# Chunked delta-rule attention, soft MoE and a gated layer in one kernel: the two halves of a chunk issued side by side

## The reference, cut to what matters

```python
# B, H, S, D = 4, 8, 768, 48
k_n = k / (norm(k) + 1e-6); state = zeros((B, H, D, D))
for t in range(S):
    y[t] = q[t] @ state
    v_old = k_n[t] @ state
    state = state + beta[t] * outer(k_n[t], v[t] - v_old)
# x = y as (B*S, H*D) = 3072 x 384
logits = x @ phi; d = softmax over tokens; c = softmax over slots
slot_out = relu((d.T @ x)[e] @ w1[e]) @ w2[e]        # 8 experts, 4 slots each
x = c @ slot_out
h = x @ w_in; out = (h * sigmoid(1.702 * h)) @ w_out  # 384 -> 2048 -> 384
```

## Time and profile before

| | us |
|---|---|
| median of 3 runs | 526.88 |
| their range | 525.96 to 527.99 |
| the profiled execution | 527.37 |
| its span, first to last instruction | 525.5 |
| TensorE busy | 456.1 (87%) |
| VectorE busy | 353.0 (67%) |
| ScalarE busy | 311.8 (59%) |
| mean granted clock of TensorE | 0.958 |

### The profile page before, as it was taken

One profiled execution on the slowest core, in us unless ns is written; L12 is line 12 of the kernel. 1 busy time (PEld: TensorE's weight loads), 2 busy tenths in 40 slices (PEclk: granted clock), 3 DMA queues, 4 the chain that ended last, 5 costly groups with the idle time before them and its releaser, 6 DMA issues.

```text
span 525.5 us, 17657 instructions
## 1 busy us (share of the span) xinstructions
PE 456.1 (87%) x7296; PEld 335.6 (64%) x7296; DVE 353.0 (67%) x1177; ACT 311.8 (59%) x711; POOL 8.2 (2%) x20
## 2 busy tenths in 40 slices
PE   7548877878777788876999599999999999999997
PEld 4434655656555566554433277788888888888885
DVE  3798999999989986422651377656565666556653
ACT  2212788788878888777230356655655655655553
POOL 2000000000000000000000000000000000000000
PEclk9557899999999999989999799999999999999999
DMA  4911344666531233699999600010100100100101
GB/s 168 374 45 41 95 124 143 190 186 186 159 100 34 78 98 111 178 212 230 335 401 412 239 0 1 7 54 1 60 0 0 60 0 0 60 0 0 62 0 61
DMA packets 24295, 59.18 MB, mean 113 GB/s; under 512 B 3104, under 2 KB 11296, under 8 KB 23840
## 3 DMA queue, kind: packets, MB, share of 16 engines
q1 hardware_dynamic: 24224, 58.16, 34.6%
HBM read 53.43 MB, written 4.72 MB: 111 GB/s over the span
## 4 chain that ended last, share of the span: by engine, by line
PE 53%; ACT 20%; DVE 16%; issue 7%; DMA 3%; ACTq 0%; DVEq 0%
PE bank L815 10%; PE bank L817 10%; PE bank L816 10%; ACT zb L827 9%; PE bank L524 6%; ACT nv L870 4%; DVE tmp L1104 4%; DVE tt L1109 4%; PE bank L793 3%; DMA wo<-in_w_out 2%; DVE g_l L1316 2%; DVE g L1313 2%; PE bank L672 2%; ACT state L827 2%; ACT g_h L827 2%
## 5 line engine op out<-in xcount | busy, mean ns | idle before, releaser
L815 PE MATMUL bank<-g_h,wo_h 128*128 128x512 f32 x288 | 113.0, 392 | 2.3 <-DVE g_l L1316 2.1
L1316 DVE TENSOR_TENSOR g_l<-g,g_h 128x512 fp32r<-128x512 f32 x96 | 66.5, 693 | 71.5 <-ACT g_h L827 71.5
L817 PE MATMUL bank<-g_l,wo_h 128*128 128x512 f32 x288 | 112.1, 389 | 0.0
L816 PE MATMUL bank<-g_h,wo_l 128*128 128x512 f32 x288 | 112.1, 389 | 0.0
L827 ACT ACTIVATE g_h<-g 128x512 fp32r<-128x512 f32 x96 | 60.7, 633 | 77.6 <-DVE g L1313 77.6
L1109 DVE TENSOR_TENSOR tt<-tt,tmp 128x110 f32<-128x110 f32 (+35 forms) x366 | 75.1, 246 | 0.2
L1104 DVE TENSOR_TENSOR tmp<-nm,tt 128x110 f32<-128x110 f32 (+35 forms) x366 | 74.8, 245 | 0.2
L1313 DVE TENSOR_TENSOR g<-bank,sig 128x512 f32<-128x512 f32 x96 | 66.2, 689 | 11.2 <-ACT sig L993 6.0
L524 PE MATMUL bank<-zb,kn 128*32 128x192 f32 (+1 forms) x736 | 40.6, 334 | 38.0 <-ACT zb L827 37.5
L827 ACT ACTIVATE zb<-bank 32x192 f32<-32x192 f32 x192 | 61.6, 321 | 6.7 <-PE bank L510 4.6
L815 PEld LDWEIGHTS bank<-g_h,wo_h 128*128 128x128 f32 x288 | 54.0, 188 | 17.5 <-issue 5.7
(11 more groups left out here) (147 smaller groups left out, 448.8 us busy)
## 6 DMA issues: line engine op xcount, KB each, us to landing
kq<-in_kq_t SPq DMA_DIRECT2D x24, 512.0 KB, 4.0
slice<-in_w SPq DMA_DIRECT2D x28, 384.0 KB, 11.2
slice<-in_w SPq DMA_DIRECT2D x12, 512.0 KB, 3.7
slice<-in_w SPq DMA_DIRECT2D x24, 256.0 KB, 5.0
vn<-in_v_nat SPq DMA_DIRECT2D x24, 192.0 KB, 3.1
out_t<-res SPq DMA_DIRECT2D x18, 256.0 KB, 2.0
kn<-in_k_nat SPq DMA_DIRECT2D x23, 192.0 KB, 2.8
win<-in_w_in SPq DMA_DIRECT2D x3, 1024.0 KB, 15.4
```

Of the source, the lines that this page charges most:

```text
L815: eng.matmul(acc[d][:], wo_h[:, f, cols], g_h[:, f % GR], start=(f == 0), stop=False)
L816: eng.matmul(acc[d][:], wo_l[:, f, cols], g_h[:, f % GR], start=False, stop=False)
L817: i = eng.matmul(acc[d][:], wo_h[:, f, cols], g_l[:, f % GR], start=False, stop=(f == NF - 1))
L1316: eng.tensor_tensor(g_l[:, f % GR], g[:, f % GR], g_h[:, f % GR].bitcast(F32), ALU.subtract).then_inc(s_gl, 1)
```

## The change

On TensorE solve 1 comes directly behind qs and the first turn, ahead of gram 0 and update 0; ks 0 of the next chunk comes behind update 1. On ScalarE z 1 comes ahead of s 0; gram_out and root go to the end of the chunk, behind nv; a chunk with turned tiles copies y behind s 1. The turned tiles are VectorE's from chunk 18, and stand behind the first portion of elimination there; the third one behind the second portion. On SP the expert loads of chunks 4 to 11 go behind those of kn and vn and wait for p_y, and the eight half loads of a chunk wait in a changed order.

```diff
+TURNS_V = NCH - 6
@@ sync
-                if CR <= c < 3 * CR:
-                    eng.wait_ge(p_z, 2 * c + 2)
-                    load_expert((c - CR) // EG, (c - CR) % EG)
...
-                    places = ((p_z, 2 * c + 1), (p_k, 2 * c + 2), (p_q, c + 1), (p_s, min(2 * c + 1, 2 * LAST)), (p_z, 2 * c + 2),
-                              (p_k, min(2 * c + 3, 2 * NCH)), (p_s, min(2 * c + 2, 2 * LAST)), (p_y, c + 1))
+                    places = ((p_z, 2 * c + 1), (p_k, 2 * c + 2), (p_q, c + 1), (p_z, 2 * c + 2), (p_s, min(2 * c + 1, 2 * LAST)),
+                              (p_s, min(2 * c + 2, 2 * LAST)), (p_k, min(2 * c + 3, 2 * NCH)), (p_y, c + 1))
...
                     load_vn(c + 3)
+                if CR <= c < 3 * CR:
+                    eng.wait_ge(p_y, c + 1)
+                    load_expert((c - CR) // EG, (c - CR) % EG)
@@ tensor
                 solve(c, 0)
                 ks(c, 1)
                 qs(c)
+                if turns[0] is not None:
+                    turn(turns[0])
+                solve(c, 1)
+                if ahead:
+                    gram(c + GA, 0)
                 if c < LAST:
                     update(c, 0)
                 else:
                     e_turned(0)
-                if ahead:
-                    gram(c + GA, 0)
-                if turns[0] is not None:
-                    turn(turns[0])
-                solve(c, 1)
-                if c < LAST:
-                    ks(c + 1, 0)
                 if ahead:
                     gram(c + GA, 1)
                 if turns[1] is not None:
                     turn(turns[1])
                 if c < LAST:
                     update(c, 1)
+                    ks(c + 1, 0)
@@ scalar
-                r, turns = c // CR + 1, TURN_AT.get(c, NO_TURNS) if c < NCH - CR else NO_TURNS
+                r, turns = c // CR + 1, TURN_AT.get(c, NO_TURNS) if c < TURNS_V else NO_TURNS
                 z_out(c, 0)
-                if c:
+                if turns[0] is not None:
+                    turn_out(eng, copy, turns[0])
+                elif c:
                     y_out(c - 1)
-                    if c - 1 + GA < NCH:
-                        gram_out(c - 1 + GA)
+                z_out(c, 1)
                 if c < LAST:
                     s_out(c, 0)
...
-                if c % CR == CR - 1 and r + 1 < NR:
-                    root(r + 1)
-                if turns[0] is not None:
-                    turn_out(eng, copy, turns[0])
-                z_out(c, 1)
                 if turns[1] is not None:
                     turn_out(eng, copy, turns[1])
                 if c < LAST:
                     s_out(c, 1)
+                if turns[0] is not None:
+                    y_out(c - 1)
+                if c < LAST:
                     scale_v(c + 1)
+                if c and c - 1 + GA < NCH:
+                    gram_out(c - 1 + GA)
+                if c % CR == CR - 1 and r + 1 < NR:
+                    root(r + 1)
@@ vector
-                r, steps, turns = c // CR + 1, ELIMINATE[c % CR], TURN_AT[c] if c >= NCH - CR else NO_TURNS
+                r, steps, turns = c // CR + 1, ELIMINATE[c % CR], TURN_AT[c] if c >= TURNS_V else NO_TURNS
...
                     if c % CR == CR - 1:
                         inverted(r)
+                if turns[0] is not None:
+                    turn_out(eng, eng.tensor_copy, turns[0])
+                if turns[1] is not None:
+                    turn_out(eng, eng.tensor_copy, turns[1])
                 if c + 1 < NCH:
                     scale_v(c + 1)
                     right_side(c + 1, 0)
                 if c and c - 1 + GA < NCH:
                     masked(c - 1 + GA)
-                if turns[1] is not None:
-                    turn_out(eng, eng.tensor_copy, turns[1])
```

More of the change, by code:

```diff
@@ L1183, in _ @@
                     slot_max(0)
-                if turns[0] is not None:
-                    turn_out(eng, eng.tensor_copy, turns[0])
                 if c == 0:
@@ L1210, in _ @@
                     c_shift(0)
-                if turns[2] is not None:
-                    turn_out(eng, eng.tensor_copy, turns[2])
                 if r < NR:
@@ L1215, in _ @@
                         eliminate(r, j)
+                if turns[2] is not None:
+                    turn_out(eng, eng.tensor_copy, turns[2])
                 if r + 1 < NR and c % CR == CR - 2:
```

## The result

The changed kernel takes 587.88 us (median of 6 runs, 585.66 to 590.27), the kernel before 527.3 beside it: a ratio of 1.116, interval 1.113 to 1.119. It is slower by 60.6 us (60.0 in the spans of the two profiled executions). The prediction had 577, 555 to 594, and slower with 0.93.

A forecast was written before the change was run, and what follows sets the result against it. VectorE's queue, nearly full with elimination, was taken to hold half 1's right side late, with ScalarE nearly full too. 33.4 + 0.3 - 1.5 + 18 = +50.2 on 527.37 gave 577.6, stated as 577 us, range 555 to 594.

The forecast's parts named there:

- Part (1): TensorE, solve 1 ahead of gram 0 and update 0: half 0's next right side starts 4.41 us after half 1's.
- Part (2): ScalarE's gram copy at the chunk's end: VectorE's mask starts at 6.63 us instead of 4.68, a wait of 1.95.
- Part (3): Sum per chunk with VectorE's elimination gaps: chunks 1 to 14 take 147.0 us against 113.6, +33.4.
- The sum of 147.0: Predicted us for chunks 1 to 14, without the slow-clock term, against 113.6 before.
- part (6): TensorE's clock falls after 4 us idle in chunks 1 to 14, 3 in chunk 15: +18 us, bounds 0 and +30.
- six tenths: Share taken of the 2.0 us a chunk that a wholly slow TensorE chain would cost: 1.2 us in 15 chunks.
- Rival B: Clock low in all of the loop: first +2.0 us in 15 chunks, then about 1 in six more; 596 us, chance 0.10.
- Part (4): Chunks 15 to 19, without mask: 43.2 us against 42.9, +0.3, bounds -3 and +4.
- The mechanism named for 18 and 19: TensorE's second turn, ahead of update 1, waits for the first's copy behind VectorE's elimination: chunks of 8.7 and 8.6 us.
- Part (5): Chunks 20 to 23: ScalarE's queue gives some 5 us less, but full DMA engines limit it: -1.5, bounds -5 and 0.
- Rivals A and C: A: TensorE's clock doesn't fall, 559.6 us, chance 0.12. C: the mask isn't what VectorE waits for, 532 us, chance 0.05.
- Rival D: Halves overlap if half 1's right side starts within 1.3 us of solve 0; VectorE's work bounds: 518 us, chance 0.05.

The follow-up runs named there:

- the run without it: Changed kernel with only the turned tiles of chunks 18 and 19 given back to ScalarE: 583.9 us, ratio 1.107.
- the one of 523.4 us: Changed kernel with gram copy and root back behind y, turned tiles on ScalarE, elimination between right sides cut to two columns or one: 523.4 us, ratio 0.994.
- the first run: Changed kernel with ScalarE's gram copy and root back directly behind y, ahead of z 1: 544.6 us, ratio 1.031.

## Why the prediction was right, and where it was off

**Direction and mechanism** were right, and the steps that carry them have their numbers. Part (1), 4.41 us to the next right side 0: 4.28. Part (2), the mask at 6.63 and 1.95 us of wait: 6.60 and 1.96. Part (3), chunk 1 at 10.17 by its sum: 10.15. The sum of 147.0 was not seen as such, since the clock was never high throughout; with filled gaps it was 150.7. That 577 fell 11 us short of the median of 587.9 (9.7 us from the sum's 577.6 to the profiled execution's 587.3) has these parts.

**The clock's term, part (6), was too small.** Over the count of 147.0, the fourteen chunks took 24.8 us more, 1.8 a chunk, where I took 1.2 and had 2.0 as the bound. The step that was off is "six tenths": I spread the slow stretch around the end of the gap, and from chunk 2 on it covered nearly all of each chain from right side 1 to the mask (7.9 to 8.9 us in chunks 2 to 13, against 6.6). Rival B's first term, and the rule of the Trainium skill, "TensorE: Matmul & The Clock Gate", section on HAM oscillation, that a loop can restart cold every time round, were nearer than my choice. The rest of rival B did not come: from chunk 17 on the clock is mostly up (mean 0.97 from 250.7 to 302.1 us). Filling the gaps took 21 of the 24.8 away. Against the 16.8 taken for these fourteen chunks the term is 8.0 of the 9.7 us short. The 4 us of idle time taken for each of them came too, but not in chunk 1, which had 1.94.

**Part (4)** gave +0.3, with 1.2 for the clock in chunk 15 in part (6), and both together measured +1.2; chunks 15 to 19 took 10.2, 9.0, 7.7, 8.5 and 8.8 for 10.0, 8.1, 7.9, 8.7 and 8.6. Chunk 16, the one furthest off, still has 3.4 us at the low clock. The mechanism named for 18 and 19 is confirmed by the run without it, -3.1 us in these two.

**Part (5)** took -1.5 for the tail; it was -0.2. From right side 1 of chunk 20 to ScalarE's first copy of w_out there are 76.6 to 76.8 us in the kernel before, the changed one, and the one of 523.4 us alike. That copy waits for its transfer; in the changed kernel:

```profile
352.36 1.48 ACT L829 ACTIVATE wo_h<-wo 128x1536 fp32r<-128x1536 f32 x1 [14.18 <-DMA wo<-in_w_out]
```

That these transfers decide is consistent with all of them; no run took transfers away, so it stays argued. SP's new order was not run by itself. The start and the third layer, which the sum left at 0, added 0.8.

**Rivals A and C** fell, A with the clock row, C with the mask's 24.4 us. **Rival D**, the halves really side by side, was rightly placed under the forecast, and its condition was right: it needs half 1's right side early. Once elimination is out of the way, order and new split together are worth 0.6%, not the 9 us (1.7%) that its sum gave. The shortest execution, 519.2 us, comes near its 518; the others, at 0.925 to 0.944 of the clock, don't.

## What to carry to other kernels

Before moving an instruction to the front of an in-order queue, look where the one it waits for stands in its own queue: solve 1 came early on TensorE, but its right side sat behind elimination on VectorE, so the order made update 0 late instead of solve 1 early. A copy that looks idle at the end of a queue, as the gram copy, may have a reader that stands in the middle of the fullest engine's. And count TensorE's idle time in a loop at the clock's price too: here gaps of 2.9 to 5.0 us went with half rate in thirteen chunks of fourteen, gaps of 1.7 to 2.9 us (the first run) in ten of fourteen, and filling the gap with dead work paid where there were some 4 us and cost where there was hardly 1.

## What the runs showed of the hardware

The granted clock depended on the loop's shape to a degree that I had underrated. In the kernel before, TensorE's gaps were under 1.3 us from 60 to 226 us, and the clock was 1.00 throughout. In the changed kernel gaps of 2.9 to 5.0 us went with 0.50 in chunks 2 to 14, and an update of 16 matmuls went from 0.84 to 1.49 us. In the first run 1.71 to 2.94 us were enough in ten chunks of fourteen; but of two gaps of 1.93 and 1.94 us (chunks 5 and 6) one left the clock up and one didn't, so the gap's length alone doesn't settle it. Ten dead matmuls a chunk took 19 us off 588.

A matmul with its start flag set changes more than its own columns. In the run with ten matmuls (start=True) only columns 384 to 511 of y's bank are written, y stands in columns 0 to 383, and the output is off by a relative error of 0.64; in the two runs with start=False it is right. The Trainium skill, "PSUM — Partial Sum Buffer", section "The four PSUM rules", says that the flag clears the written-marks of the whole bank in the 32-partition quadrants that the matmul writes, so that a later accumulating matmul overwrites there. These kernels agree: pz would overwrite the part from qs.
